# Five copies of the turned weights moved from ScalarE to VectorE, with the first batch's routing set between them

## The reference

```python
# attention: q, k, v are [2 batches, 8 heads, 576, 64]
scores = q @ k.T / 8
kth = 32nd largest score of each row
scores = where(scores >= kth, scores, -1e9)
attn = softmax(scores)
x = (attn @ v) laid out as [1152 tokens, 512]
# mixture of experts: 8 experts, capacity 288 rows each
logits = x @ w_gate                       # 1152 x 8
expert = argmax(logits); gate = softmax(logits)[expert]
pos = number of earlier tokens that chose the same expert   # dropped from 288 on
disp[expert, pos] = x
h = relu(disp @ w1[e]); y = h @ w2[e]     # w1 512 x 1024, w2 1024 x 512
out[token] = gate * y[expert, pos]
```

## Time and profile before

| what | value |
|---|---|
| time, median of 3 runs | 464.2 us (463.43 to 465.82) |
| the profiled execution's own time | 464.91 us |
| its span, first to last instruction | 463.2 us |
| PE busy | 405.7 us, 88% of the span |
| PEld busy | 344.4 us, 74% |
| DVE busy | 287.6 us, 62% |
| ACT busy | 242.2 us, 52% |
| POOL busy | 240.2 us, 52% |
| mean granted clock of TensorE | 0.962 of full speed |

### The profile page before, as it was taken

One profiled execution on the slowest core, in us unless ns is written; L12 is line 12 of the kernel. 1 busy time (PEld: TensorE's weight loads), 2 busy tenths in 40 slices (PEclk: granted clock), 3 DMA queues, 4 the chain that ended last, 5 costly groups with the idle time before them and its releaser, 6 DMA issues.

```text
span 463.2 us, 8672 instructions
## 1 busy us (share of the span) xinstructions
PE 405.7 (88%) x2753; PEld 344.4 (74%) x2753; DVE 287.6 (62%) x1397; ACT 242.2 (52%) x428; POOL 240.2 (52%) x229
## 2 busy tenths in 40 slices
PE   2986768989698798896899999899999999999993
PEld 1653336877487687685788889796999999999771
DVE  2699799999899999989999964501011122121210
ACT  2233358987887888877688996041312121222320
POOL 4054459889788888898799776031101010120310
PEclk9999957999999999999798999999999999999997
DMA  4220204031041133003110104859999785867500
GB/s 102 53 51 2 51 1 143 2 110 43 19 144 28 40 105 116 2 15 105 26 70 2 27 1 132 335 178 367 339 327 343 261 290 192 278 218 247 188 22 19
DMA packets 53538, 57.85 MB, mean 125 GB/s; under 512 B 34286, under 2 KB 34286, under 8 KB 53488
## 3 DMA queue, kind: packets, MB, share of 16 engines
q1 hardware_dynamic: 51344, 52.51, 35.9%
q0 software_dynamic: 2144, 4.73, 2.8%
HBM read 45.39 MB, written 13.79 MB: 128 GB/s over the span
## 4 chain that ended last, share of the span: by engine, by line
PE 36%; POOL 4%; ACT 3%; issue 3%; DMA 3%; DVE 2%; SPq 0%; DVEq 0%; POOLq 0%; ACTq 0%
PE ps_s L863 14%; PE ps_s L881 11%; PE ps_o L654 3%; PE ps_o L838 3%; DMA scores<-in_moe_w_dram 2%; PE ps_t L626 2%; POOL probs L477 2%; POOL rest L472 1%; ACT pT L958 1%; ACT probs L951 1%; PE ps_s L680 1%; PE ps_o L819 1%; PE ps_t L807 1%; DMA dispatched<-x,r_slot 1%; POOL dispatched L485 1%
## 5 line engine op out<-in xcount | busy, mean ns | idle before, releaser
L472 POOL TENSOR_TENSOR rest<-below,scores 128x576 f32<-128x576 f32 x69 | 96.1, 1411 | 50.6 <-DVE below L1121 50.6
L654 PE MATMUL ps_o<-v_aug,pT 128*128 128x128 f32 (+2 forms) x800 | 103.1, 279 | 0.0
L477 POOL TENSOR_TENSOR probs<-scores,probs 128x576 f32<-128x576 f32 x72 | 101.6, 1429 | 2.4 <-ACT probs L945 2.4
L654 PEld LDWEIGHTS ps_o<-v_aug,pT 128*128 128x128 f32 (+1 forms) x800 | 96.5, 186 | 1.7 <-issue 1.6
L1022 ACT ACTIVATE scores<-ps_s 128x288 f32<-128x288 f32 x64 | 26.3, 411 | 104.3 <-PE ps_s L863 104.3
L1056 DVE MAX8 cand<-scores 128x8 f32<-128x96 f32 x432 | 72.5, 243 | 12.2 <-ACT scores L919 12.2
L626 PE MATMUL ps_t<-ident,probs 128*128 128x128 f32 (+1 forms) x360 | 56.1, 289 | 21.9 <-ACT pT L958 15.9
L863 PE MATMUL ps_s<-scores 128*128 128x192 f32 (+3 forms) x448 | 66.6, 306 | 0.7 <-DMA scores<-in_moe_w_dram 0.7
L626 PEld LDWEIGHTS ps_t<-ident,probs 128*128 128x128 f32 (+1 forms) x360 | 38.2, 139 | 37.4 <-issue 20.1
L863 PEld LDWEIGHTS ps_s<-scores 128*128 128x128 f32 x448 | 64.3, 191 | 2.0 <-issue 2.0
L919 ACT ACTIVATE scores<-ps_s 128x576 f32<-128x576 f32 x72 | 46.0, 646 | 37.6 <-PE ps_s L599 20.1
(11 more groups left out here) (133 smaller groups left out, 394.1 us busy)
## 6 DMA issues: line engine op xcount, KB each, us to landing
w_sb<-in_moe_w_dram SPq DMA_DIRECT2D x9, 2048.0 KB, 12.7
scores<-in_moe_w_dram SPq DMA_DIRECT2D x7, 2048.0 KB, 10.1
dispatched<-empty SPq DMA_DIRECT2D x18, 257.0 KB, 3.6
scores<-dispatched SPq DMA_DIRECT2D x21, 192.8 KB, 4.0
out_dram<-empty SPq DMA_DIRECT2D x9, 256.0 KB, 3.0
q_nat<-in_q_dram SPq DMA_DIRECT2D x16, 128.0 KB, 2.2
k_nat<-in_k_dram SPq DMA_DIRECT2D x16, 128.0 KB, 2.3
v_aug<-in_v_dram SPq DMA_DIRECT2D x16, 128.0 KB, 2.3
```

The costliest lines, as they stand in the source:

```text
L472: nc.gpsimd.tensor_tensor(rest[:, n % 3, :], below[:, n % 3, :], score_tile(n), ALU.mult).then_inc(rest_ready, 1)
L477: nc.gpsimd.tensor_tensor(probs[:, n % PROBS, :], score_tile(n), probs[:, n % PROBS, :], ALU.subtract).then_inc(masked_ready, 1)
L654: last = nc.tensor.matmul(dst, lhs, v_aug[:, g % 2, c, h, 0:width], start=(c == 0), stop=(c == TT - 1))
```

## The change

The copies C(63), C(65), C(67), C(69) and C(71) leave ScalarE's list and go into VectorE's, where there is now a function of the same name. `router_exponentials(0)` moves by two steps, from s = 90 to s = 92. On VectorE `normalise(PAIRS - 2, 1)` now comes ahead of `choose_experts(0)`, and a wait for constants ahead of `choose_experts(0)` is gone.

```diff
+    SHARED = ALL - TILES
 ...
-                if 0 <= p - 3 < ALL:
+                if 0 <= p - 3 < ALL and (p - 3 < SHARED or (p - 3 - SHARED) % 2 == 1):
                     copy_pT(p - 3)
-                if s == ALL + CHOSEN - 2:
+                if s == ALL + CHOSEN:
                     router_exponentials(0)
 ...
+            def copy_pT(n):
+
+                dve.wait_ge(pT_in_psum, n + 1)
+                dve.wait_ge(pv_done, n - 1)
+                nc.vector.tensor_copy(pT[:, n % 2, :], ps_t[:, 0:TT * P]).then_inc(pT_copied, 1)
 ...
             normalise(PAIRS - 2, 0)
+            copy_pT(SHARED)
             recheck(CHECKS - 1, count_bad(CHECKS - 1))
-            dve.wait_ge(consts_ready, 12)
+            copy_pT(SHARED + 2)
+            normalise(PAIRS - 2, 1)
             choose_experts(0)
-            normalise(PAIRS - 2, 1)
+            copy_pT(SHARED + 4)
             assign_slots(0)
+            copy_pT(SHARED + 6)
             choose_lead()
             normalise(PAIRS - 1, 0)
+            copy_pT(SHARED + 8)
             lift_lead()
             dve.wait_ge(masked_ready, 2 * HELD)
             mark_slots(0)
```

## The result

| | before | changed |
|---|---|---|
| median of 20 runs, us | 464.95 (463.15 to 467.51) | 467.04 (465.06 to 469.87) |
| ratio to before, 95% interval | 1 | 1.0049 (1.0034 to 1.0065) |
| the profiled execution, us | 464.91 | 466.34 |
| its span, us | 463.2 | 464.4 |

By the ratio the change costs 2.3 us (1.6 to 3.0) of 465. I had forecast +0.8 us and a time of 465.0 with a range up to 466.85. Even with the median of before 0.75 us higher over 20 runs than over the 3 that I had, the step is more than twice mine.

A forecast was written before the change was run, and what follows sets the result against it. ScalarE bounds the chain until T(67), then TensorE until VectorE's last normalise. With -0.1 us at T(68) and +0.9 in the tail, +0.8 on a median of 464.2 gives 465.0 us, range 463.2 to 466.85.

The forecast's parts named there:

- The step that failed: In choose_experts(0) on VectorE: r_hot gets in beside mask 71, T(68) starts at about 279.15, -0.1 us at T(68).
- The second rival: At choose_experts(0): r_hot is held too by mask 71 until 279.43, T(68) at 280.45, total +2.15 us, 466.35; chance 0.14.
- the third, the clock: Rival: idle TensorE around 277.7 to 279.15 and at 290 loses its clock, 1.7 to 3.4 us more; chance 0.1.
- The tail: After C(71) on VectorE: lift_lead, mark_slots(0) and the logits' sum delay the last normalise from 290.18 to 291.05, +0.9 us.
- The lead load: At choose_lead behind C(69): lead expert's weights asked for 2.8 us later, free with over 5 us of slack.
- ScalarE's relief: On ScalarE up to T(67): five copies fewer, 2.9 us of work, so T(67) starts 1.3 us earlier.
- The copy: On VectorE: one copy of 640 columns out of PSUM takes 0.82 us, bounds 0.69 to 0.98.
- The router's exponentials: On ScalarE, moved behind exp(68): 0.13 us of work, and the move costs nothing by itself.
- the sum: Whole kernel: -0.1 us at T(68) and +0.9 us in the tail, +0.8 us in all.

The follow-up runs named there:

- e7: The changed kernel with choose_lead moved ahead of C(69), so the lead expert's weights are asked for earlier: ratio to before 1.0015 (0.9996 to 1.0034).
- e3: The changed kernel with r_hot, r_dif and the second r_pick reading their second input from PSUM, one reduction more: ratio to before 0.9974 (0.9950 to 0.9999).

## Why the prediction was wrong

**The step that failed** is the one that I had as level: "`r_hot` comes at 278.05, level with mask 71; if it gets in, it is done at 278.2." The times around it came as worked out. With 1.16 us added, the two traces' offset at T(63), excess(71) started at 277.17 (forecast 277.18), mask 70 ended at 277.96 (277.97), `r_pick` was held to 278.02 (278.0), mask 71 started at 278.01 (278.02) and `r_hot` at 278.05 (278.05). So the two were not level: the mask was first by 0.04 us, and by 0.03 in my own numbers. What I had read from the rows, that such an operation waits until the mask is through, then holds `r_hot` until the end of mask 71. I let it in against that. `r_hot` was held in all seven profiles that have this order of work, and in each it started 0.04 to 0.08 us behind mask 71. So T(68) is +1.17 us and not -0.1. The second rival had that price (+1.25) and a chance of 0.14.

**The second failing step** is that this rival and the third, the clock, were held to exclude each other. The hold makes the wait before the ranks 1.7 us long, and after it the clock fell in three of five profiles. Together they cost 2.1 us on average. My price for a fall was 1.7 to 3.4 us, for which I gave no working but the 2 us from the row at half clock; it measured 1.5 to 1.6.

**The tail** was mis-sized: +0.9 forecast, +0.5 measured. From T(71) to `normalise` I had 3.8 us and it took 3.44. C(71)'s successor starts 0.74 us behind it, not 0.85, and the list up to the `normalise` takes 1.95, not 2.2, since I had counted the end of its last row, which its successor overlaps, and the small gap ahead of an instruction that had waited.

**The lead load** was mis-sized as well: asked for 2.8 us later by the forecast, 5.6 us later behind T(63) in the trace (19.99 for 14.43). Of this, 2.7 us are the delay at T(68) and the fall of the clock, 1.17 and 1.52. The verdict that it is free held in the trace.

**Right**: ScalarE's relief won 1.29 us by T(67) (forecast 1.3). The copy takes 0.81 to 0.83 us (0.82). It is not held by masks, and r_dif and r_pick are (1.18 and 1.30 us). C(63), C(65) and C(69) cost nothing. The router's exponentials cost nothing. The rule that GpSimd shares its SBUF interfaces with an instruction of two SBUF inputs (the Trainium skill, GPSIMD Engine Reference, Key points) held for `r_hot` as well, and when its second input was moved to PSUM the same instruction took 0.20 us beside a mask. That the late lead load is free has the doubt that e7 leaves.

**What I had not in the sum**: 0.73 us of PE's wait for the second expert's weights, which takes up delays of the chain (-0.90 in the table).

Sum for an average execution, from the traces: 1.17 + 0.9 + 0.5 + 0.2 - 0.9 - 0.1 = 1.8 us, within the measured 1.6 to 3.0. The middle of that interval is 0.5 higher; that is not accounted for.

## What to carry to other kernels

Work taken off a busy engine comes back where the receiving engine has other duties in order: here a copy behind a router's chain, which the same relief then held up, since it closed the gaps between GpSimd's masks. Where two engines come out level in a forecast, go by the order that the numbers give, however small the difference, and price the other order too: 0.04 us decided over 1.2 here; and don't give a hold and its consequence (an idle TensorE, and its clock) chances as if only one could come. If a small operation of VectorE with two SBUF inputs must run beside GpSimd, one input in PSUM kept it from being held here.

## What the runs showed of the hardware

- **TensorE's clock after a wait.** In the stretch from T(63) to P1 it fell after waits of 1.71 or 1.72 us in three of five profiles, of 1.83 and 1.84 in two of two, of 1.87 in three of three, and not after 1.78 (once) nor 1.60 to 1.63 (six times). But it also fell once after waits of 1.06 and 0.43 us close together (e3), which at the same place left it alone in e7. So the length of the last wait does not decide it by itself. Earlier in the kernel waits of up to 2.96 us were followed by full clock in some profiles and half in others. A fall lasted 3 to 4 us, and from T(68) to x it cost 1.5 to 1.6 us.
- **The hold** ends with the mask, and a second instruction 0.03 us behind the first is held by the next mask in full, 1.4 us (seven profiles). Reductions (0.18 us), copies from PSUM and operations with one input in PSUM went through beside masks. Two SBUF inputs are not the only case that is held: before the change two operations with one SBUF input and a constant took 1.15 and 1.09 us, to within 0.03 us of the ends of masks 69 (277.33) and 71 (281.18), where the first took 0.17 for the second batch with no mask running.

```profile
276.21 1.15 DVE L1225 TENSOR_SCALAR r_sum<-r_sum 128x5 f32<-128x5 f32 x1
...
280.12 1.09 DVE L1240 TENSOR_SCALAR r_drop<-r_pos 128x5 f32<-128x5 f32 x1
```

- **A load asked for later landed sooner after its issue**: the second expert's weights took 10.1 us issued at 310.0 before, 8.7 us issued at 311.9 in the changed kernel, so that 1.9 us of lateness became 0.5. What makes it sooner was not tried.
